# Attention stage of a fused attention and mixture-of-experts kernel: last products with v a step sooner, first transposes a step later, the sinks' rows of v in one load

## What is computed

```python
def _attn_ref(q, k, v, n_sink, window):
    scores = scale * np.matmul(q, k.transpose(0, 1, 3, 2))
    is_sink = pos[None, :] < n_sink
    rel = pos[:, None] - pos[None, :]
    keep = is_sink | ((rel >= 0) & (rel < window))
    scores = np.where(keep, scores, -1e9)
    a = np.exp(scores - np.max(scores, axis=-1, keepdims=True))
    a = a / (np.sum(a, axis=-1, keepdims=True) + 1e-09)
    return np.matmul(a, v)
```

## The kernel before

| step | PE after the scores | DVE after `mask_max` | ACT after `exp_tile` |
|---|---|---|---|
| 0 | turn(p-1, 1) | normalise(p-1, 2), rest_x(p-2), copy(p-1, 1) | round_x(p-2), copy(p-1, 1), scale(p-1, 2) |
| 1 | pv(p-1, 0) | | |
| 2 | turn(p-1, 2) | normalise(p, 0), copy(p-1, 2) | copy(p-1, 2), scale(p, 0) |
| 3 | turn_sinks(p-1), pv(p-1, 1) | rest_v_sinks(p-1) | copy_sinkT(p-1) |
| 4 | turn(p, 0) | normalise(p, 1), copy(p, 0) | copy(p, 0), scale(p, 1) |
| 5 | pv(p-1, 2), pv_sinks(p-1) | | |

## Time and profile before

### The profile page before, as it was taken

One profiled execution on the slowest core, in us unless ns is written; L12 is line 12 of the kernel. 1 busy time (PEld: TensorE's weight loads), 2 busy tenths in 40 slices (PEclk: granted clock), 3 DMA queues, 4 the chain that ended last, 5 costly groups with the idle time before them and its releaser, 6 DMA issues.

```text
span 1251.3 us, 18785 instructions
## 1 busy us (share of the span) xinstructions
PE 1236.2 (99%) x6446; PEld 1097.3 (88%) x6446; DVE 691.7 (55%) x1348; ACT 365.1 (29%) x832; POOL 535.7 (43%) x625
## 2 busy tenths in 40 slices
PE   7999999999999999999999999999999999999998
PEld 4558899989988999999999999999999999999997
DVE  7895734356665555555555555555555555555554
ACT  7884634312233222222222222222222222222221
POOL 7772315644444444444444444444444444444440
PEclk9999999999999999999999999999999999999999
DMA  6440000111110111111111111111111111111102
GB/s 204 156 149 18 1 1 1 34 35 34 34 35 28 38 36 36 34 34 34 34 34 34 34 34 34 34 34 34 34 34 34 34 34 34 34 34 34 35 18 101
DMA packets 57264, 53.13 MB, mean 42 GB/s; under 512 B 4352, under 2 KB 44544, under 8 KB 57216
## 3 DMA queue, kind: packets, MB, share of 16 engines
q1 hardware_dynamic: 56928, 52.19, 13.1%
q10 hardware_dynamic: 288, 0.33, 0.1%
HBM read 49.35 MB, written 3.15 MB: 42 GB/s over the span
## 4 chain that ended last, share of the span: by engine, by line
PE 95%; ACT 2%; DVE 2%; DMA 1%; issue 1%; SPq 0%; DVEq 0%; ACTq 0%
PE ps L797 30%; PE ps L798 30%; PE ps L799 30%; PE ps L722 2%; PE ps L766 1%; PE ps L742 1%; PE ps L847 1%; ACT probs L1042 1%; ACT acc L1218 1%; DVE probs L1270 1%; DMA k_sb<-kT 0%; PE ps L977 0%; DVE xw L1303 0%; ACT xw L1066 0%; DMA q_sb<-qT 0%
## 5 line engine op out<-in xcount | busy, mean ns | idle before, releaser
L1528 DVE SCALAR_TENSOR_TENSOR acc<-ps,gate_now,acc 128x512 f32<-128x512 f32 x336 | 252.1, 750 | 166.2 <-PE ps L799 162.0
L797 PE MATMUL ps<-ring 128*128 128x512 f32 x768 | 300.6, 391 | 0.0
L798 PE MATMUL ps<-ring 128*128 128x512 f32 x768 | 299.8, 390 | 0.0
L799 PE MATMUL ps<-ring 128*128 128x512 f32 x768 | 299.2, 390 | 0.0
L1200 ACT ACTIVATE sums<-ps 128x384 f32<-128x384 f32 x192 | 94.4, 492 | 597.8 <-PE ps L799 597.8
L1504 DVE TENSOR_TENSOR sums<-ps,sums 128x384 f32<-128x384 f32 x192 | 106.9, 557 | 158.2 <-ACT sums L1200 106.9
L799 PEld LDWEIGHTS ps<-ring 128*128 128x128 f32 x768 | 144.3, 188 | 30.9
L797 PEld LDWEIGHTS ps<-ring 128*128 128x128 f32 x768 | 144.2, 188 | 27.9 <-DVE acc L1524 0.4
L798 PEld LDWEIGHTS ps<-ring 128*128 128x128 f32 x768 | 144.2, 188 | 25.8
L642 POOL TENSOR_TENSOR w_raw<-w_raw 128x256 f32<-128x256 f32 x32 | 23.7, 741 | 321.3 <-PE ps L799 321.3
L797 PE MATMUL ps<-xw,ring 128*128 128x384 f32 x448 | 152.5, 340 | 0.3 <-ACT sums L1200 0.2
(11 more groups left out here) (148 smaller groups left out, 1765.2 us busy)
## 6 DMA issues: line engine op xcount, KB each, us to landing
w_in<-w_exp SPq DMA_DIRECT2D x64, 256.0 KB, 3.2
w_raw<-w_exp SPq DMA_DIRECT2D x64, 128.0 KB, 2.8
w_raw<-w_exp SPq DMA_DIRECT2D x32, 256.0 KB, 3.2
v_sb<-v SPq DMA_DIRECT2D x16, 192.0 KB
out<-acc SPq DMA_DIRECT2D x12, 256.0 KB, 2.0
q_sb<-qT SPq DMA_DIRECT2D x7, 384.0 KB, 4.4
k_sb<-kT SPq DMA_DIRECT2D x7, 384.0 KB, 4.9
k_sb<-kT SPq DMA_DIRECT2D x9, 256.0 KB, 5.7
```

Source lines behind the costliest of these rows:

```text
L797: pe.matmul(o, ws[0], xs[0], start=first, stop=False, skip_group_check=True)
L798: pe.matmul(o, ws[0], xs[1], start=False, stop=False, skip_group_check=True)
L799: return pe.matmul(o, ws[1], xs[0], start=False, stop=last, skip_group_check=True)
L1528: dve.scalar_tensor_tensor(out=acc[:, T, :], in0=y_bank(u, T), scalar=gate_now[:, T:T + 1], in1=acc[:, T, :], op0=ALU.mult, op1=ALU.add).t ...
```

## The change

Four things are done together.

- PE: `pv(p-1, 2)` and `pv_sinks(p-1)` move from step 5 to step 4, and `turn(p, 0)` from step 4 to step 5. The copies of its two banks move to step 5 as well, on ACT and DVE.
- `round_x` and `rest_x` of pair p-1 move from step 0 of pair p+1 to step 5 of pair p, ahead of these copies.
- The sinks' rows of v are loaded for all pairs at once, by 6 DMAs in place of 48, and rounded and split once, both on POOL (`split_v_sinks`), in pair 0 between lay_sinks(1) and the rounding of segment 0. The split on DVE in every pair is gone.
- The memset of that buffer, now four times as wide, moves behind the masks, and SP waits for it after the loads of v and of segment 0 of pair 0.

```diff
-        v_sink = sb("v_sink", [SINK_ROWS, 2, P], F32, in_a)
-        v_sink_r = sb("v_sink_r", [SINK_ROWS, 2, P], F32R, in_a)
+        v_sink = sb("v_sink", [SINK_ROWS, PAIRS, P], F32, in_a)
+        v_sink_r = sb("v_sink_r", [SINK_ROWS, PAIRS, P], F32R, in_a)
...
             def load_v(p, h):
                 sp.dma_start(v_sb[:, p % 2, h, :], v[p, h]).then_inc(v_loaded[p % 2], 16)
+
+            def load_v_sinks(h):
                 for row in (0, 32, 64):
                     row += h * NS
-                    sp.dma_start(v_sink[row:row + NS, p % 2, h * DH:(h + 1) * DH],
-                                 v[p, h, 0:NS, 0:DH]).then_inc(v_loaded[p % 2], 16)
+                    sp.dma_start(v_sink[row:row + NS, :, h * DH:(h + 1) * DH],
+                                 v[:, h, 0:NS, 0:DH].rearrange("p n d -> n p d")).then_inc(v_sinks_loaded, 16)
...
-            sp.wait_ge(consts, 2)
             for h in range(2):
                 load_v(0, h)
             load_segments(0)
+            sp.wait_ge(v_sinks_clear, 1)
+            for h in range(2):
+                load_v_sinks(h)
...
-            pool.memset(v_sink[:, :], 0.0).then_inc(consts, 1)
...
+            pool.memset(v_sink[:, :, :], 0.0).then_inc(v_sinks_clear, 1)
             pool.memset(sink_cols[:, :, :].bitcast(F32), 0.0).then_inc(sinks_hi, 1)
...
+            def split_v_sinks():
+                pool.wait_ge(v_sinks_loaded, 96)
+                pool.tensor_scalar(v_sink_r[:, :, :], v_sink[:, :, :], 1.0, 0.0,
                                    ALU.mult, ALU.add).then_inc(v_sinks_hi, 1)
+                pool.wait_ge(v_sinks_hi, 1)
+                low = v_sink_r[64:SINK_ROWS, :, :]
+                pool.tensor_tensor(low, v_sink[64:SINK_ROWS, :, :], low.bitcast(F32),
+                                   ALU.subtract).then_inc(v_sinks_split, 1)
+                pool.wait_ge(v_sinks_split, 1)
...
                 if p == 0:
+                    split_v_sinks()
                     round_segments(0)
                     rest_w_in(0)
...
                 split_sinks(p)
-                round_v_sinks(p)
...
-                if t == 4:
-                    if p == 0:
-                        pe.wait_ge(consts, 3)
-                    turn(p, 0)
-                if t == 5 and p > 0:
+                if t == 4 and p > 0:
                     pv(p - 1, 2)
                     pv_sinks(p - 1)
+                if t == 5:
+                    if p == 0:
+                        pe.wait_ge(consts, 2)
+                    turn(p, 0)
...
-                if t == 0 and p > 1:
-                    round_x(p - 2)
...
                 if t == 4:
+                    scale_probs(p, 1)
+                if t == 5:
+                    if p > 0:
+                        round_x(p - 1)
                     copy_pT(p, 0, 0)
-                    scale_probs(p, 1)
...
-                    if p > 1:
-                        rest_x(p - 2)
                     copy_pT(p - 1, 1, 1)
...
-                if t == 3 and p > 0:
-                    rest_v_sinks(p - 1)
                 if t == 4:
                     normalise(p, 1)
+                if t == 5:
+                    if p > 0:
+                        rest_x(p - 1)
                     copy_pT(p, 0, 1)
```

More of the change, by code:

```diff
@@ L219, in solu_moe @@
         sinks_hi, sinks_split = sem("sinks_hi"), sem("sinks_split")
+        v_sinks_clear, v_sinks_loaded = sem("v_sinks_clear"), sem("v_sinks_loaded")
         v_sinks_hi, v_sinks_split = sem("v_sinks_hi"), sem("v_sinks_split")
@@ L503, in _ @@
             pool.memset(mask1[:, 0:NS], 0.0).then_inc(masks, 1)
+            pool.memset(v_sink[:, :, :], 0.0).then_inc(v_sinks_clear, 1)
             pool.memset(sink_cols[:, :, :].bitcast(F32), 0.0).then_inc(sinks_hi, 1)
-            pool.wait_ge(consts, 2)
+            pool.wait_ge(consts, 1)
             pool.affine_select(out=ident[:, :], in_=ident[:, :], compare_op=ALU.not_equal, fill=1.0,
@@ L758, in pv @@
                 if b == 0:
-                    pe.wait_ge(v_loaded[p % 2], 128 * (p // 2 + 1))
+                    pe.wait_ge(v_loaded[p % 2], 32 * (p // 2 + 1))
                     if p > 0:
@@ L771, in pv_sinks @@
                 pe.wait_ge(*copied(p, SINK_USE))
-                pe.wait_ge(v_sinks_split, p + 1)
-                pe.matmul(x_psum(2, QT), v_sink_r[:, p % 2, :], sinkT[:, :],
+                pe.wait_ge(v_sinks_split, 1)
+                pe.matmul(x_psum(2, QT), v_sink_r[:, p, :], sinkT[:, :],
                           start=False, stop=True, skip_group_check=True).then_inc(x_full, 1)
@@ L835, in _ @@
             back(PAIRS, 3)
-            back(PAIRS, 5)
+            back(PAIRS, 4)
             def turn_ln(b, f):
@@ L1091, in _ @@
                     act.wait_ge(small_loaded, 32)
-                    act.wait_ge(consts, 5)
+                    act.wait_ge(consts, 4)
                     act.activation(wg[:, :, WG_AT:WG_AT + EXPERTS], wg_raw[:, :, :], ACT.Copy).then_inc(wg_ready, 1)
@@ L1292, in copy_pT @@
                                 t_bank(p, use)[:, 0:(n1 - n0) * P]).then_inc(pT_dve, 1)
-            def rest_v_sinks(p):
-                dve.wait_ge(v_sinks_hi, p + 1)
-                low = v_sink_r[64:SINK_ROWS, p % 2, :]
-                dve.tensor_tensor(low, v_sink[64:SINK_ROWS, p % 2, :], low.bitcast(F32),
-                                  ALU.subtract).then_inc(v_sinks_split, 1)
             def rest_x(p):
@@ L1403, in _ @@
             copy_pT(PAIRS - 1, 2, 1)
-            rest_v_sinks(PAIRS - 1)
             solu(1)
```

6 lines of the change are left out of this document (removed).

## The result

The changed kernel takes 1258.21 us at the median of six runs (1257.93 to 1259.36); the kernel before took 1253.64 beside it, also six runs (1252.11 to 1255.93). The ratio is 1.0044, with a 95% interval of 1.0034 to 1.0054: slower, 4.6 us. The forecast was 1258.7, slower by more than 0.2%; it started from a median of 1254.23, so against the 1253.64 measured beside it the same +4.5 would be 1258.1. The profiled execution of the changed kernel took 1257.96 us with a span of 1256.2, 4.9 more than the span before.

What follows compares the result with a forecast made beforehand. The prediction took three engines waiting for each other in fixed order, none full, as the bound. Start +2.8 and ring +1.7 gave +4.5 on 1253.09, 1257.6, or 1258.7 as a median; range 1252.5 to 1261.5.

Steps and rivals of the forecast that it cites:

- The bound: Whole kernel: TensorE alone fills the 1157.42 us after attention, so only the first 94 us count.
- The ring after, 11.89, +1.7: Cycle through VectorE and ScalarE per pair: 7.54 + 0.83 + 3.52 = 11.89 against 11.55, +1.7 us over five pairs.
- the bound of 11.4 to 11.5 for a ring without POOL: Changed pair cycle: 11.4 to 11.5 us if POOL does not work beside VectorE's 260-wide normalisation instruction.
- PE's wait moves to the copy and to the scores: In each pair: PE's wait, 4.0 us in all before, moves from pv(p, 0) to turn(p, 1) and the scores.
- The start, +2.8: Pairs 0 to 2: POOL's added v-sinks work puts step 1's mask in pair 2 at 31.15 instead of 28.35.
- have landed by 11.81: Pair 0: the sinks' rows of v must land by 11.81; no wait counted, 1 us possible.
- what costs nothing: Items put at no cost: the wider memset (about 1 us), 42 fewer DMA issues, the end after pair 7.
- The load comes last: Start of pair 2: its q and k loads, not turn(0, 2), set PE's scores at 27.2; were they quicker, +2.2.
- The 4.5 carries to the end unchanged: From step 1's mask in pair 7 to h1_half, PE works without a gap before and after: difference 0.
- The ring didn't open: Rival on the pair cycle: early round_x lets PE's 10.75 set the pair, -4.0, giving 1253.0 us; chance 0.10.
- The "faster" rival: Whole kernel: faster than before by more than 0.2%, 2.5 us; chance 0.11.
- The rival of late loads: Start: sinks' DMAs land after 11.81, or later segments push POOL into pair 2's ring: +1 to +3, 1260 to 1262; chance 0.13.

Runs made afterwards that it cites:

- e1: The kernel before with the new order of steps alone, the sinks' v still loaded, rounded and split for each pair: 1258.00 us, ratio 1.0046.
- e2: The changed kernel with the old order of steps, so only the sinks' v done once for all pairs: 1255.58 us, ratio 1.0026 against the kernel before.
- e6: The changed kernel with rest_x put back behind the normalisation of batch 2 in the next pair: 1257.95 us, ratio 1.0035 against the kernel before.
- e4: The changed kernel with POOL's wide memset held back until VectorE has laid the sinks' key columns: 1258.21 us, ratio 1.0047 against the kernel before.
- g1: e4 with the six loads of the sinks' v issued ahead of pair 0's v and first segments: 1257.06 us, ratio 1.0030 against the kernel before.
- g2: g1 with head 0's four transposes of turn(0, 2) issued five times, keeping PE busy: 1257.18 us, against g1's 1257.06.
- e5: The changed kernel with head 0's four transposes of turn(0, 2) issued five times, keeping PE busy while it waits for POOL: 1257.27 us in one run.
- f2: The kernel before with only the split of the sinks' v moved from VectorE to POOL, pair by pair: 1250.10 us, ratio 0.9980.
- f3: f2 with ScalarE's round_x also moved ahead of the exps of step 0, rest_x left in place: 1248.49 us, ratio 0.9969 against the kernel before.
- e3: The changed kernel with the sinks' v rounding and split placed later on POOL, behind split_sinks of pair 0: 1255.53 us, ratio 1.0030 against the kernel before.

## Why the prediction held, point by point

**The number.** The ring's mechanism carried the forecast. That the sum came within 0.4 us of the spans (+4.9 against +4.5) is partly luck: the start was 1.1 us more than forecast, and the tail (-0.48) and the part behind h1_half (-0.2), both put at nothing, took 0.7 of that back.

**The bound.** That only the start of h1_half counts was right: 1157.2 us stand behind it in both.

**The ring after, 11.89, +1.7.** Right in the sum, +1.68, and in each leg: 7.51 against 7.54, 0.83 against 0.83, 3.50 against 3.52; idle times of 1.63 and 1.32 against 1.8 and 1.4. The legs add up to 11.84, the length of the common pair; the mean is 11.89 only because pair 3 takes 12.07, with VectorE's 128x128 normalise at 0.53 instead of 0.29. And the forecast set a common pair after against a mean before that two long pairs raise. A common pair grew by 0.45, not by 0.34, and the long ones by less (pair 2 shrank by 0.04). That these cancel to 0.01 us is luck. e1 and e2 confirm the two halves of the trade. The split of the sinks' v was put at 0.50 and its gap; e2 measured 0.45 a pair in the mean, 0.33 in a common one. e6 shows the part of rest_x's new place, 0.21 to 0.26 a pair. What the prediction undercounted shows in e1: in the new order that split falls deeper into POOL's subtraction, 0.88 instead of 0.50, so the order alone costs more than the +0.34 plus 0.5 of its terms. That didn't matter here, since the split is gone. One row behind a bound was misread: at 21.57 POOL does work beside the 260-wide instruction of 0.42 us (its normalise until 21.85, L565 from 21.80). Without POOL beside it the same instruction takes 0.36 (e4, at 12.92), so the bound of 11.4 to 11.5 for a ring without POOL stands on the wrong row; no run shows that ring.

**PE's wait moves to the copy and to the scores.** Right, 2.3 us in five waits ahead of turn(p, 1), and the masks.

**The start, +2.8.** The mechanism was right, the size wrong: +3.94. The term for POOL held: 3.56 us from the start of the rounding at 13.00 to the next instruction at 16.56, forecast 3.5, and so did the queue behind it. (The terms behind 27.2 add up to 3.89, so the forecast mask is 31.1 by its own sum and not 31.15.) VectorE was held 2.31 us, forecast about 2.5, on the instruction behind the one named (L1292, not L1285, the former L1278). The step that failed is "have landed by 11.81" with POOL free at that time. Two prices are missing. First, under "what costs nothing" the wider memset was checked against its followers on POOL only, not against VectorE: it lies beside VectorE's copies and these stand until POOL's run of memsets ends at 6.34 (e4: 0.25 without it). Second, the loads of the sinks land late, at 13.3 in e4, where the forecast took 11.4 from a single load of one row of the trace, allowing 1 us more at worst; in the changed kernel, where they were issued 0.14 earlier, they are there when POOL comes to them at 13.00, and the first delay hides them. g1 takes both away, and the mask stands at 31.12, forecast 31.15. That agreement is partly luck. In g1 the lower clock is in it, in g2 it isn't, and the mask comes at 30.63, because the keys are there at 26.65, 0.55 before the forecast 27.2.

**"The load comes last".** Wrong in the changed kernel, right in e5 and g2. PE had no wait for keys since its clock was at half for some 3 us after it had stood for POOL, 0.75 us of the start. The prediction had read the wait for POOL and not asked what the clock does behind it. Together, by g1: 2.77 of the 3.94 are there without the two holds and 1.17 are theirs; inside the 2.77, g2 puts 0.49 down to the clock.

**"The 4.5 carries to the end unchanged".** Wrong by 0.48, to the good. Both kernels have the same instructions on PE between step 5's scores and h1_half, in another order. PE before, then after; then f2, which has the old order with the split off VectorE, and e1, which has the new order with the split still there:

```profile
91.26 0.87 PE L742 MATMUL ps<-ident,probs 128*128 128x128 f32 x6
92.06 1.30 PE L766 MATMUL ps<-pT,v_sb 128*64 128x256 f32 x12
93.29 0.50 PE L773 MATMUL ps<-sinkT,v_sink_r 72*128 72x512 f32 x1
93.88 0.47 PE L797 MATMUL ps<-xw 128*128 128x512 f32 x1
```
```profile
96.87 1.30 PE L772 MATMUL ps<-pT,v_sb 128*64 128x256 f32 x12
98.10 0.50 PE L779 MATMUL ps<-sinkT,v_sink_r 72*128 72x512 f32 x1
98.44 0.82 PE L748 MATMUL ps<-ident,probs 128*128 128x128 f32 x6
99.02 0.48 PE L803 MATMUL ps<-xw 128*128 128x512 f32 x1
```
```profile
90.83 0.50 PE L778 MATMUL ps<-sinkT,v_sink_r 72*128 72x512 f32 x1
91.17 0.40 PE L802 MATMUL ps<-xw 128*128 128x512 f32 x1
```
```profile
98.89 0.47 PE L797 MATMUL ps<-xw 128*128 128x512 f32 x1 [0.41 <-DVE a_stat L1271]
```

It is 2.62 us to h1_half before (91.26 to 93.88) and 2.15 after (96.87 to 99.02). Two things make the 0.47. The sinks' product is followed after 0.34 instead of 0.59. That isn't the order, for f2 and e2, with the old order, show 0.34 and 0.33. h1_half also waits until VectorE has read the last scores, in e1 for 0.41 us as the bracket says; before, VectorE's last mask is done at 93.74 and h1_half starts at 93.88, in f2 it is done at 90.95 and h1_half starts at 91.17, right behind the sinks' product. So by these rows 0.25 is a wait for VectorE that goes with its split, a gap where the prediction said there was none. The other 0.22 goes with the order: the six transposes are followed after 0.58 instead of 0.80. Why was not tried.

**The rivals.** The ring didn't open (11.89), but not because it can't: f3 opens it to 10.78. The "faster" rival needed a cheap subtraction on 8 rows, and it took 2.35. The Trainium skill (GPSIMD Engine Reference, "Architecture") gives each GpSimd core 16 partitions of its own, from which the prediction took that few rows save nothing; the trace agrees, 2.35 us for 8x1024 beside 1.27 for 128x512. The rival of late loads was half true: they land at 13.3, 1.5 us late in e4, and in the changed kernel behind another delay. Its total of 1260 to 1262 didn't come.

**The rule on the shared port.** The Trainium skill (SBUF — State Buffer, "SBUF: two separate sides") has GpSimd and a VectorE instruction in a two-port mode, or with two SBUF inputs, exclude each other for one whole instruction. Three rows agree: 2.31 us at 14.31, 2.24 us in e3, and 0.88 in e1, each ending within 0.15 us of POOL's subtraction. The row at 4.00 goes further: there VectorE stands not for one memset of 0.95 us, but over five instructions of POOL.

## What to carry to other kernels

Work that is done once instead of in every round is dear where it lands in the start, with other engines queued behind it: here it made the start 3.9 us longer, 3.6 us of it POOL's own work, and took 0.45 us off each of five pairs, and the same split done pair by pair on the same engine gave the gain without the price. Add up a ring of two in-order engines from start to start before moving a step: here the early rounding paid (f3) only where the partner didn't wait for it with other work behind. And check a longer instruction on POOL against every instruction of VectorE that can meet it, setup code too.

## What the runs showed of the hardware

- Beside POOL's memset of 72x1024 two VectorE copies of 128x20 took 2.39 us, until POOL's run of memsets and one affine select ended at 6.34 (copies' end 6.39). It doesn't hang on the memset being first: it starts 0.06 us ahead of the copies in the changed kernel and 0.11 and 0.17 behind them in e2 and e6, and in all three the copies end at 6.39. With the memset behind the copies they took 0.25 (e4, g1). Why the copies don't get in between two of POOL's instructions stays open.
- POOL's subtraction takes 2.35 us for 8x1024 and 0.45 for 8x128, that is (2.35 - 0.45) / 896 = 2.1 ns a column and 0.18 us fixed; by these, 512 columns take 1.27 us, which is what the 128x512 one takes. Between 8 and 128 rows these show no difference.
- PE idle for 2.17 us at a granted clock of 1.00 was followed by a clock of 0.50 (1.2 GHz) from about 22 to 25 in the changed kernel, and from about 21 to 27 in e6, after 2.19. In e2 it was 0.50 from 21 to about 27.5 after waits of 1.73 and 1.52 within 5 us. With the last wait cut to 0.44 in e5 it stayed at 1.00, as it did after single waits of 1.27 (before) and 1.41 (e3).
- Six loads of 8 KB in 256-byte pieces, issued at 6.3 to 8.4 behind those of v and of the segments, landed at 13.3 (e4). Issued at 5.2 to 7.3, ahead of them (g1), they had landed by 11.8.
